# A linear-attention recurrence on one core: its turns and logits in 64x64 tile matmuls, and one loop body for all 24 units

## The reference, cut to what matters

```python
B, H, S, D = 4, 8, 768, 48
for t in range(S):                                   # linear attention
    cur = einsum('bhd,bhe->bhde', u[None] * kt, vt)
    y[:, :, t] = einsum('bhd,bhde->bhe', rt, state + cur)
    state = w[None, :, :, None] * state + einsum('bhd,bhe->bhde', kt, vt)
x = y.transpose(0, 2, 1, 3).reshape(3072, 384)
logits = x @ phi                                     # 32 slots
slot_input = softmax_over_tokens(logits).T @ x       # then 8 experts: relu(. @ w1) @ w2
x = softmax_over_slots(logits) @ slot_out
h = maximum(x @ w_in, 0); out = (h * h) @ w_out      # 384 -> 2048 -> 384
```

## Time and profile before

| | us |
|---|---|
| Runs: median of 3 (lowest to highest) | 427.72 (427.62 to 429.63) |
| The profiled execution, its own time | 427.09 |
| Its span, first to last instruction | 425.4 |
| First PE instruction (L991) | 15.12 |
| Start of the loop over chunks | 44.1 |
| First `gather` after the recurrence | 142.02 |

### The profile page before, as it was taken

The page is one execution under the profiler, slowest core; times in us unless marked ns, Lnnn a source line. Parts: engine busy times, 40 slices in busy tenths (PEclk is TensorE's granted clock), DMA queues, the critical chain, the costliest instruction groups (busy, mean ns, idle before and its releaser), DMA issues.

```text
span 425.4 us, 12269 instructions
## 1 busy us (share of the span) xinstructions
PE 382.4 (90%) x4984; PEld 334.9 (79%) x4984; DVE 243.4 (57%) x403; ACT 199.2 (47%) x360; POOL 53.9 (13%) x83
## 2 busy tenths in 40 slices
PE   0387798999988889966999999999999999999997
PEld 0267687988976323535999999999999999999996
DVE  7243546777744470149755665656575666566653
ACT  3142355666643110354445555655555565556452
POOL 3223123424400011048000000000000000000000
PEclk9997889999999889988999999999999999999999
DMA  2398748998740999960000200200020010002002
GB/s 47 96 313 261 213 115 251 273 300 273 233 168 18 378 373 372 406 239 0 2 1 2 74 2 0 72 3 0 0 74 0 0 41 33 0 0 74 2 0 74
DMA packets 29021, 50.85 MB, mean 120 GB/s; under 512 B 3776, under 2 KB 23232, under 8 KB 28608
## 3 DMA queue, kind: packets, MB, share of 16 engines
q1 hardware_dynamic: 28992, 50.44, 36.5%
HBM read 45.71 MB, written 4.72 MB: 119 GB/s over the span
## 4 chain that ended last, share of the span: by engine, by line
PE 88%; issue 4%; DVE 4%; SPq 1%; ACT 1%; DMA 1%; POOL 0%; DVEq 0%; POOLq 0%; ACTq 0%
PE out_ps L1195 48%; PE score_ps L882 7%; PE h_ps L1173 5%; PE y_ps L905 4%; PE kt_ps L870 3%; PE y_ps L922 3%; PE inc_ps L893 3%; PE wide L1111 3%; PE x_ps L864 3%; PE wide L1136 2%; PE x_ps L850 1%; PE x_ps L857 1%; PE wide L1063 1%; DVE act_lo L829 1%; DMA recept<-in_rk_t 1%
## 5 line engine op out<-in xcount | busy, mean ns | idle before, releaser
L1195 PE MATMUL out_ps<-w_hi,act_hi 128*128 128x384 f32 x384 | 130.9, 341 | 5.4 <-DVE act_lo L829 4.9
L1195 PE MATMUL out_ps<-w_lo,act_hi 128*128 128x384 f32 x384 | 130.6, 340 | 0.0
L1195 PE MATMUL out_ps<-w_hi,act_lo 128*128 128x384 f32 x384 | 130.5, 340 | 0.0
L824 DVE TENSOR_TENSOR act<-relu_h 128x512 f32<-128x512 f32 x96 | 68.7, 715 | 78.9 <-ACT relu_h L600 78.9
L600 ACT ACTIVATE relu_h<-h_ps 128x512 f32<-128x512 f32 x96 | 57.4, 598 | 101.5 <-PE h_ps L1173 100.9
L1195 PEld LDWEIGHTS out_ps<-w_hi,act_hi 128*128 128x128 f32 x384 | 72.4, 189 | 6.6 <-ACT act_hi L603 3.8
L1195 PEld LDWEIGHTS out_ps<-w_lo,act_hi 128*128 128x128 f32 x384 | 72.6, 189 | 4.3
L1195 PEld LDWEIGHTS out_ps<-w_hi,act_lo 128*128 128x128 f32 x384 | 72.5, 189 | 0.0
L829 DVE TENSOR_TENSOR act_lo<-act,act_hi 128x512 fp32r<-128x512 f32 x96 | 68.4, 713 | 4.6 <-ACT act_hi L603 1.0
L603 ACT ACTIVATE act_hi<-relu_h 128x512 fp32r<-128x512 f32 x96 | 60.9, 634 | 3.9
L1173 PE MATMUL h_ps<-mix_t,gin 128*128 (+1 forms) x96 | 38.7, 406 | 0.0
(11 more groups left out here) (157 smaller groups left out, 392.3 us busy)
## 6 DMA issues: line engine op xcount, KB each, us to landing
w_sb<-in_w SPq DMA_DIRECT2D x21, 512.0 KB, 5.0
w_room<-in_w SPq DMA_DIRECT2D x4, 1536.0 KB, 12.5
keys_in<-in_rkv_n SPq DMA_DIRECT2D x24, 192.0 KB, 4.3
recept<-in_rk_t SPq DMA_DIRECT2D x48, 96.0 KB, 3.6
values<-in_rkv_n SPq DMA_DIRECT2D x24, 192.0 KB, 3.9
out_dram<-y_sb SPq DMA_DIRECT2D x5, 768.0 KB, 3.6
w_x<-in_w SPq DMA_DIRECT2D x2, 1536.0 KB, 13.8
w_w<-in_w SPq DMA_DIRECT2D x4, 768.0 KB, 11.4
```

The costliest lines, as they stand in the source:

```text
L824: nc.vector.tensor_tensor(act[f % 2][:, :], relu_h[f % 2][:, :], relu_h[f % 2][:, :], ALU.mult).then_inc(act_done, 1)
L1195: last = nc.tensor.matmul(out_ps[t][:, 0:DM], a[f % 4][:, tok], w[:, f], start=(f == 0 and i == 0), stop=(f == NF - 1 and i == 2))
```

## The change

What it does, part by part:

- `turn_x` and `turn_keys` are no longer transposes of 128x128 but 16 small matmuls each, with an identity as the moving operand: 64x48 and 48x64.
- `pair_logits`, the copy `logits_t` and `token_logits` go. `logit_parts` takes their place: 64 matmuls at hp = 1 that give the logits token-major in the two banks of `turn_ps`, and DVE adds the two banks into `logits` (`add_logits`).
- `x_ps` and `kt_ps`, one bank each, become the one buffer `turn_ps` of two banks. It is used in turn by the key turn, the x turn and the logits.
- PE's loop runs over all six chunks, with an order of its own: own(n-1), scores(n), key turn(n+1), carried(n) and state(n+1), x turn(n-1). Chunk 0 and chunk 5 have no code of their own any more. So that the first unit fits the pattern, own(-1), the x turn(-1) and the first logits work on buffers set to zero, and counters start at 1 or 2.
- DVE's and ACT's orders follow: DVE does mask(n), advance(n+1), scale(n+2); ACT does keep_x(n-2), copy_y(n-1), keep_keys(n+1), scale_bonus(n+1). POOL's `keep_state` now waits for a transfer of values too, and PE's state step waits for `keep_state`.
- The start is rearranged. DVE clears two `recept` buffers and not six (POOL clears the rest) and makes the turned powers before the query powers and before it waits for the second transfer of queries. The first values are loaded before the parameters, the keys have three buffers and not two, and the `w1` pieces begin three units later.
- Behind the loop DVE takes the maximum of the earlier logits one unit sooner, and its two memsets of `wide` stand after the last subtraction and not before it.

```diff
-K_BUFS = 2
+K_BUFS = 3
...
             def keep_state(n):
-                pool.wait_ge(state_next_done, n + 1)
-                pool.wait_ge(carried_done, n + 1)
-                nc.gpsimd.tensor_copy(state_a[0:PAIR, n % HP], state_next[0:PAIR, n % HP]).then_inc(state_a_ready, 1)
+                c, hp = n // HP, n % HP
+                if n + 2 < UNITS:
+                    pool.wait_ge(values_in[(n + 2) % V_BUFS], 16 * ((n + 2) // V_BUFS + 1))
+                pool.wait_ge(carried_done, n + 2)
+                if c < CH - 1:
+                    pool.wait_ge(state_next_done, n + 1)
+                    nc.gpsimd.tensor_copy(state_a[0:PAIR, hp], state_next[0:PAIR, hp]).then_inc(state_a_ready, 1)
...
+            def add_logits(c):
+                ve.wait_ge(logit_mm, c + 2)
+                halves = turn_ps[:, :].rearrange("p (r q) -> p q r", r=2)[:, 0:B * SLOTS]
+                nc.vector.reduce_sum(logits[:, c * B:(c + 1) * B, :].rearrange("p b s -> p (b s)"), halves, AX.X
+                                     ).then_inc(lg_free, 1)
...
-            def token_logits(bank):
+            def logit_parts(pairs):
+                for hp in pairs:
+                    for b in range(B):
+                        for r, s in TILES_64:
+                            at = BANK * r + SLOTS * b
+                            last = nc.tensor.matmul(turn_ps[HALVES[s], at:at + SLOTS], x_t[HEAD_ROWS[r], hp, b, HALVES[s]],
+                                                    phi_sb[HEAD_ROWS[r], b % 2, hp], start=(hp == 0 and b == 0), stop=True,
+                                                    skip_group_check=True)
...
-                    last = nc.tensor.transpose(bank[:, P * b:P * b + PAIR], x_t[0:PAIR, hp, b], ident[0:PAIR, 0:PAIR])
+                    for r, s in TILES_64:
+                        at = BANK * r + D * b
+                        last = nc.tensor.matmul(bank[HALVES[s], at:at + D], x_t[HEAD_ROWS[r], hp, b, HALVES[s]],
+                                                ident[HEAD_ROWS[r], HEAD_ROWS[r]], start=True, stop=True)
...
-            with pe.Fori(1, CH - 1) as c:
-                chunk(c, False)
-            chunk(CH - 1, True)
+            with pe.Fori(0, CH) as c:
                 for hp in range(HP):
                     n = c * HP + hp
+                    own_step(n - 1, (hp - 1) % HP)
                     if hp == 1:
+                        pe.wait_ge(x_done, n + 1)
+                        settled()
+                        logit_parts(range(HP)).then_inc(logit_mm, 1)
                     scores_step(n, hp)
                     if hp == 1:
                         pe.wait_ge(lg_free, c + 1)
+                    keys_step(n + 1, (hp + 1) % HP)
+                    carried_step(n, hp)
+                    state_step(n + 1, (hp + 1) % HP)
+                    carried_rest(n, hp)
+                    turn_step(n - 1, (hp - 1) % HP)
```

More of the change, by code:

```diff
@@ L96, in program @@
     keys = [place(f"keys{i}", [P, B, P]) for i in range(2)]
-    keys_n = [place(f"keys_n{i}", [P, B, 2, SECOND]) for i in range(HP)]
+    keys_n = [place(f"keys_n{i}", [P, B, 2, D]) for i in range(HP)]
     keys_in = [place(f"keys_in{i}", [P, B, 2 * D]) for i in range(K_BUFS)]
@@ L122, in program @@
     w_pow = place("w_pow", [P, HP, SUB + 1], at=w1_at + 4 * (NW - 1) * KD * FE)
[L123 removed]
+    kn_powt = place("kn_powt", [P, HP, SUB], at=place.end)
     mask = place("mask", [P, P], U32, at=place.end)
@@ L403, in _ @@
                 chained(nc.gpsimd.tensor_copy(mask_sub[rows, :].bitcast(F32), mask[rows, rows].bitcast(F32)))
+            for i in range(2, R_BUFS):
+                nc.gpsimd.memset(recept[i][SUB // 2:SUB], 0.0).then_inc(back_cleared, 1)
+            pool.wait_ge(back_cleared, R_BUFS - 2)
+            nc.gpsimd.memset(values[HP - 1][:, :, :], 0.0).then_inc(carried_done, 1)
+            for hp in range(HP):
+                if hp == HP - 1:
+                    pool.wait_ge(values_in[1], 16)
+                nc.gpsimd.memset(state_a[:, hp], 0.0).then_inc(state_a_ready, 1)
             def turned_keys(n):
@@ L869, in turn_keys @@
                 for b in range(B):
-                    last = nc.tensor.transpose(kt_ps[:, P * b:P * (b + 1)],
-                                               keys_n[i][:, b].rearrange("p h d -> p (h d)"), ident[:, :])
+                    for s, h in TILES_64:
+                        at = BANK * s + SUB * b
+                        last = nc.tensor.matmul(turn_ps[HEAD_ROWS[h], at:at + SUB], keys_n[i][HALVES[s], b, h],
+                                                ident_sub[HALVES[s], :], start=True, stop=True)
                 last.then_inc(kt_mm, 1)
@@ L892, in unit_state @@
                             at = BANK * s + D * b
-                            last = nc.tensor.matmul(inc_ps[rows, at:at + D], keys_n[hp][part, b, h, 0:D],
+                            last = nc.tensor.matmul(inc_ps[rows, at:at + D], keys_n[hp][part, b, h],
                                                     values[hp][part, b, D * h:D * (h + 1)], start=True, stop=True)
@@ L907, in carried, with unit_carried, unit_own @@
                                         skip_group_check=True)
-            def unit_carried(hp, half, first):
+            def unit_carried(hp, half):
                 for b in range(B):
-                    s = (b + half) % 2
-                    if s or not first:
-                        for h in range(2):
-                            last = carried(hp, b, h, s)
+                    for h in range(2):
+                        last = carried(hp, b, h, (b + half) % 2)
                 last.then_inc(carried_done if half else carried_half, 1)
-            def unit_own(hp, first):
+            def unit_own(hp):
                 def own(b, h, s):
@@ L988, in _, with carried_rest @@
+            def carried_rest(n, hp):
+                pe.wait_ge(carried_half, n + 1)
+                settled()
+                unit_carried(hp, 1)
             pe.wait_ge(const_step, IDENT)
             pe.wait_ge(pow_t_done, 1)
-            for p in range(HP):
-                last = nc.tensor.transpose(x_ps[:, P * p:P * p + PAIR], kn_powt[0:PAIR, p].rearrange("p s t -> p (s t)"),
-                                           ident[0:PAIR, 0:PAIR])
+            pe.wait_ge(ps_cleared, 1)
+            for hp in range(HP):
+                for r, s in TILES_64:
+                    at = BANK * r + D * hp
+                    last = nc.tensor.matmul(turn_ps[HALVES[s], at:at + D], kn_powt[HEAD_ROWS[r], hp],
+                                            ident[HEAD_ROWS[r], HEAD_ROWS[r]], start=True, stop=True)
@@ new lines, in _ @@
+                    carried_rest(n, hp)
+                    turn_step(n - 1, (hp - 1) % HP)
+            pe.wait_ge(pmax_done, 1)
+            nc.tensor.transpose(wide[1][0:SLOTS, 0:P], slot_t[:, 1, :], ident[:, :]).then_inc(pmax_t_done, 1)
+            own_step(UNITS - 1, HP - 1)
+            pe.wait_ge(x_done, UNITS + 1)
+            logit_parts(range(HP - 1))
+            pe.wait_ge(y_copied, UNITS + 1)
+            logit_parts((HP - 1,)).then_inc(logit_mm, 1)
+            turn_x(HP - 1, score_ps)
```

351 lines of the change are left out of this document (155 added, 196 removed).

## The result

The changed kernel takes **445.2 us** (median of 4 runs: 444.39, 445.05, 445.33, 469.57), the kernel before 428.7 beside it (427.62 to 431.08). The ratio, which leaves the slow run of 469.57 out, is 1.037, 95% interval 1.031 to 1.043: slower by 3.7%. The forecast was 420, faster; the time lies inside the range of 410 to 466, the sign was wrong. The profiled execution took 445.05 us, its span is 443.3.

The account below looks back on a forecast made before the run. PE was taken to bound the kernel (88% of 425.4 us). From 427.1, own(23) 6.7 earlier and 0.5 off the tail gave 419.9, with 0.6 to the median 420.5, say 420; range 410 to 466.

Parts of the forecast that it names:

- rival A: PE's loop body stays loaded after its first pass: 420 us, own range 411 to 426, chance 53%.
- rival C: PE's loop code is loaded anew in each pass, places reused in loading order: 533 us, or some 510; chance 15%.
- B: Loop body does not quite fit; each of five branches back waits for one or two packet loads: 457 us, chance 19%.
- on entering the eighth: At the loop body's end, PE entering its eighth code packet makes a ninth be loaded ahead; no separate size.
- Start: Before the loop: POOL's first key scaling at 13.5 instead of 17.00, bounds 10 and 17; first loop matmuls at about 16.
- Chunk 0: The loop's first pass: seven code packets at 4.8 us each plus 0.5, ending at 50.1.
- Chunks 1 to 5: The loop's later passes: 15.7 us a chunk against 15.87 before, bounds 14.9 and 16.4; five take 78.5.
- The logits: The 128 new logit matmuls in each chunk: 1.7 us plus 0.25 of waiting, saving 0.3 a chunk.
- the upper bound: New logit matmuls with 32 columns cost at most 0.26 / 16 each, 2.1 us a chunk.
- The tight place at the mask: In each unit, own needs its mask 2.63 after scores begin; PE has 2.8 us of work there, 0.2 to spare.
- Own(23): The last unit's own step, at the loop's end, starts at 128.6 instead of 135.35: -6.7.
- The tail: Behind the loop: first gather some 1.7 us nearer to own(23), the two memsets cost about 1.2; net -0.5.

Follow-up runs that it names:

- the delay by increments: Semaphore increments on PE added ahead of the changed kernel's loop: 558.08 us with 240, 557.79 us with 248, 524.51 and 527.31 us with 40.
- the two kernels of the tail: Seven-packet version (x turns again four transposes) with memsets behind the second maximum: 415.14 us; also early-maximum matmul ahead of logits, exponential and first memset earlier: 415.34 us.
- at 86 instructions: Changed kernel with 8 more small matmuls ahead of the loop, so 86 body instructions lie in its eighth packet: 445.08 and 471.34 us.
- at 94: Changed kernel with 94 body instructions in its eighth packet: by 40 increments 524.51 and 527.31 us, by 10 more small matmuls 530.25 and 531.18 us.

## Why the prediction was wrong

**The step that failed** is the choice of rival A, "the body stays loaded", at 53%: the sum has no term for a pass loaded anew, and one such pass cost 23.2 us. Its working stated the condition correctly: the body touches eight packets, a ninth is loaded ahead, it decides from room for eight or less. I had put weight on the old kernel's keeping six and a seventh, which says nothing of an eighth and a ninth. The room is eight. The Trainium skill, "Runtime: NRT & Kernel Launch", section "Instruction fetch mechanics", has 128 KiB in 16 KiB blocks used as a FIFO; the runs agree with that (nine touched, five reloads; seven touched, none).

**What happens then** is rival C's mechanism, not B's: the places are reused in the order of loading, so one packet too many costs the whole pass. C's price, 22.7 us per pass, was right (23.2 for one; 20.8 to 22.3 per pass of five), and the kernels that reload every time took 524 to 533, with the delay by increments taken off, where C said 533. What no rival had is that the ninth isn't asked for in every pass: I took "on entering the eighth". Here it was asked for at about one branch back of five, and the changed kernel landed at 422 + 23. The time inside the range is chance.

**The terms of the sum, without the reload** (421.8 against 419.9):

- *Start.* First key scaling at 12.50, forecast 13.5. SP was done with phi at 8.04 (forecast 7.9) and issued the values at 8.09; they landed by 10.7, 2.6 us later, where I had taken 4 from the median of all values.
- *Chunk 0.* Seven packets, as forecast. Own of the next pass at 47.02 instead of 50.1, and 1.5 us more in its first unit (51.92 - 47.02 = 4.90 against 3.36 later), at a low clock: 48.6 in effect, 1.5 better.
- *Chunks 1 to 5.* A unit without logits 61.07 - 57.70 = 3.37, forecast 3.39. The logits 2.07 and a wait of 0.31, forecast 1.7 and 0.25. So 32 moving columns took as long per record (2.07 us / 128 = 16 ns) as the 64 of a carried half (0.26 / 16): the upper bound was right. With the branch, 0.3 instead of 0.2, a pass is 16.18, forecast 15.7; five make 2.4 more, and a chunk is dearer than the old 15.87 by 0.3. The tight place at the mask didn't show: PE is never idle between two owns of a clean pass outside the logits.
- *Own(23)*, without the reload, 129.4: forecast 128.6.
- *The tail* +0.6 instead of -0.5. The memsets cost 1.25, forecast 1.2; the gather came 0.6 further from own(23) and not 1.7 nearer, since the sum had no term for a packet border behind the loop (1.06 us) and for the lower clock there. From the matmul behind `slot_in` to the end of the span it was 1.1 shorter than before (274.65 against 275.72), for which I have no cause.

So the 5.3 us between 427.1 and 421.8 come from the start and from code that is loaded once and not three times; the small matmuls gave nothing of it.

```profile
12.50 2.90 POOL L431 TENSOR_TENSOR keys_n<-keys_in,kn_pow 128x384 f32<-128x384 f32 x3
```

```profile
57.70 0.66 PE L949 MATMUL y_ps<-scores,values 64*48 64x64 f32 x32
61.07 0.66 PE L949 MATMUL y_ps<-scores,values 64*48 64x64 f32 x32
```

## What to carry to other kernels

Count a loop body's code in packets of 256 instructions on the engine that bounds it, with the place where it starts, before its matmuls are counted in time: seven packets were safe in 22 runs of 22 (the two kernels of the tail among them), eight cost 0 to 110 us by where the border fell, nine cost a reload of 22 us in every pass. A rewriting in smaller tiles that is neutral in PE time isn't neutral in code: 16 small matmuls for four transposes were 56 instructions more for each unit, and taking that one turn back made the change a gain of 3% (0.970 and 0.974). And where a chain in a tail is shortened, ask for the transfers that run beside it: here they were 1 to 2 us behind.

## What the runs showed of the hardware

- PE kept eight packets of 16 KB (none was loaded between 48 and 81 us), and a ninth cost the whole pass, nine packets and 23.2 us. How far PE is in the eighth when it branches decides: at 86 instructions one or two reloads in five, at 94 five of five, with the same code otherwise. What asks for the ninth in one pass and not in another isn't known.
- A body that by the count began on a border, with the branch's label two instructions ahead of it, was reloaded in every pass (557.79 us, 63 packets), like one that began 8 instructions ahead of the border. The count is good to a few instructions only.
- A semaphore increment on PE took 0.15 us: 170 of them between the powers' turn and the first key turn took 25.48 us. 64 small matmuls (256 instructions) fitted into the same idle time: the first key turn began at 14.72 and not at 13.63, and what it waited for was POOL's keys, not PE.
- A reloaded pass cost clock too: its mean granted clock was 0.68, against 0.96 and 0.97 in the stages beside it, with gaps of up to 6.07 us in which PE stood still.
